# A linear attention and two feed-forward networks on one core: weight loads issued by ScalarE, attention rows moved within SBUF, a wait put off, empty products left out

## The reference

```python
# q, k, v, a_re, a_im: (B=4, H=8, S=768, D=48), float32
mag = sqrt(a_re**2 + a_im**2)
scale = minimum(mag, 0.999) / (mag + 1e-6)
for t in range(S):                       # a complex decay per head and column, a real state update
    S_re, S_im = ar*S_re - ai*S_im + k[t] (x) v[t],  ar*S_im + ai*S_re
    y[t] = q[t] @ S_re
x = y as (3072 tokens, 384)
xn = x / sqrt(mean(x*x) + 1e-6) * rms_g  # first network
x = (silu(xn @ w_gate) * (xn @ w_val)) @ w_out        # 384 -> 1536 -> 384
h = x @ w_in                             # second network
out = softplus(h) @ w_out2                            # 384 -> 2048 -> 384
```

## Time and profile before

| | |
|---|---|
| median of 3 runs | 1174.2 us (1171.81 to 1175.09) |
| the profiled execution | 1175.1 us, its span 1173.4 us |
| TensorE clock granted, mean | 0.997 of full speed |
| TensorE busy | 1074.7 us, 92% of the span |
| VectorE busy | 701.8 us, 60% |
| ScalarE busy | 679.3 us, 58% |
| GpSimd busy | 290.2 us, 25% |
| HBM read, written | 67.97 MB, 29.24 MB |
| `rows_scratch<-pk`, 24 stores of 771.0 KB | median 4.9 us to landing |
| `mm<-rows_scratch`, 96 loads of 192.8 KB | median 4.5 us to landing |
| `a_in`, 24 loads of 384.0 KB | median 4.9 us to landing |
| `kq_in`, 24 loads of 384.0 KB | median 5.9 us to landing |

### The profile page before, as it was taken

How to read it: one execution, slowest core, us unless ns; L and a number is a source line. 1 busy time by engine, 2 the same in 40 slices (tenths; PEclk the granted TensorE clock), 3 DMA queues, 4 the chain that set the end, 5 groups by cost and what they waited for, 6 DMA issues and landing times.

```text
span 1173.4 us, 17259 instructions
## 1 busy us (share of the span) xinstructions
PE 1074.7 (92%) x5495; PEld 913.2 (78%) x5495; DVE 701.8 (60%) x2227; ACT 679.3 (58%) x1217; POOL 290.2 (25%) x260
## 2 busy tenths in 40 slices
PE   0456689999999999999999999989999999999997
PEld 0456678888888888888888878878888888888886
DVE  7798959999999999999999211212221313122211
ACT  5566646555555565665554333466666667676664
POOL 2211211111111111111111116733333333333332
PEclk9999999999999999999999999989999999999999
DMA  4988853433343443334332303320100101010000
GB/s 114 208 206 216 189 128 88 115 89 88 89 137 100 106 132 107 88 88 116 88 89 75 101 1 122 119 70 1 52 3 1 55 0 54 0 54 0 27 1 28
DMA packets 69051, 98.15 MB, mean 84 GB/s; under 512 B 5232, under 2 KB 58864, under 8 KB 68976
## 3 DMA queue, kind: packets, MB, share of 16 engines
q1 hardware_dynamic: 63792, 90.15, 27.0%
q0 software_dynamic: 5184, 7.08, 3.9%
HBM read 67.97 MB, written 29.24 MB: 83 GB/s over the span
## 4 chain that ended last, share of the span: by engine, by line
PE 34%; issue 26%; DVE 11%; DMA 11%; POOL 10%; ACT 6%; SPq 1%; POOLq 0%; DVEq 0%; ACTq 0%
PE gbank L1488 16%; POOL pl L556 10%; PE ybank L1488 10%; DMA rows_scratch<-pk 5%; DMA mm<-rows_scratch 4%; DVE prep L882 3%; PE sbank L1505 2%; DVE pk L882 2%; PE xbank L1517 2%; PE xbank L1516 1%; PE xbank L1520 1%; ACT L730 1%; PE xbank L1496 1%; DMA ytile<-in_w 1%; DVE state L1066 1%
## 5 line engine op out<-in xcount | busy, mean ns | idle before, releaser
L1488 PE MATMUL gbank<-xh,slab 128*128 128x512 f32 x1296 | 404.3, 393 | 1.5 <-ACT xh L641 1.5
L1488 PE MATMUL ybank<-ph,slab 128*128 128x512 f32 x1020 | 319.6, 395 | 4.8 <-ACT ytile L678 3.9
L1488 PEld LDWEIGHTS gbank<-xh,slab 128*128 128x128 f32 x1296 | 241.5, 189 | 50.2 <-ACT xh L641 1.7
L1488 PE MATMUL gbank<-xl,slab 128*128 128x512 f32 x648 | 253.3, 391 | 0.0
L1488 PEld LDWEIGHTS ybank<-ph,slab 128*128 128x128 f32 x1020 | 189.3, 189 | 42.9 <-issue 5.6
L531 POOL TENSOR_TENSOR pl<-hid,ph 128x512 fp32r<-128x512 f32 x72 | 99.7, 1384 | 461.4 <-ACT ph L671 461.4
L1488 PE MATMUL ybank<-pl,slab 128*128 128x512 f32 x510 | 199.6, 391 | 0.0
L556 POOL TENSOR_TENSOR pl<-hid,ph 128x512 fp32r<-128x512 f32 x96 | 125.6, 1309 | 268.0 <-ACT ph L817 268.0
L1368 DVE SCALAR_TENSOR_TENSOR hid<-gbank,hid 128x512 f32<-128x512 f32 x72 | 49.7, 691 | 214.4 <-ACT hid L808 214.4
L1488 PEld LDWEIGHTS gbank<-xl,slab 128*128 128x128 f32 x648 | 122.0, 188 | 26.2
L1488 PEld LDWEIGHTS ybank<-pl,slab 128*128 128x128 f32 x510 | 96.2, 189 | 20.8
(11 more groups left out here) (155 smaller groups left out, 1604.0 us busy)
## 6 DMA issues: line engine op xcount, KB each, us to landing
rows_scratch<-pk SPq DMA_DIRECT2D x24, 771.0 KB, 4.9
mm<-rows_scratch SPq DMA_DIRECT2D x96, 192.8 KB, 4.5
a_in<-in_a SPq DMA_DIRECT2D x24, 384.0 KB, 4.9
kq_in<-in_kq SPq DMA_DIRECT2D x24, 384.0 KB, 5.9
ytile<-in_w SPq DMA_DIRECT2D x36, 192.0 KB, 4.7
slab<-in_w POOLq DMA_DIRECT2D x36, 192.0 KB, 5.7
prep<-in_w SPq DMA_DIRECT2D x32, 192.0 KB, 2.5
y_scratch<-ytile SPq DMA_DIRECT2D x7, 768.0 KB, 5.4
```

What stands on the lines that cost most here:

```text
L1488: last = pe.matmul(out, slab[:, slot + part, cols], x, start=f, stop=l)
```

## The change

1. **Rows within SBUF.** `rows_scratch`, `store_pk` and `load_mm` go. `move_rows(m, hf)` copies `pk` to `mm` by DMA from SBUF to SBUF: for each part z and each piece of a head that lies in one block of partitions, a DMA of 48, 32 or 16 rows of 257 numbers. A half has 5 pieces, so 10 DMAs, and a unit 20 (at most 48 x 257 numbers, 49 KB, each) instead of 1 + 4. `pk` is free when both halves have landed.
2. **SyncE's order.** In a lead step: ten moves, `load_v`, ten moves, `load_a(n+1)`, `load_kq(n)`. In a tile step `load_v` and ten moves, `load_a(n+1)`, ten moves, `load_kq(n)`.
3. **The first network's weight loads** are issued by ScalarE: those of block 0 at its start, and in `w1_hi(f)`, behind each kind's two copies, that kind of block f+1.
4. **ScalarE's order.** `w1_hi` of a lead step's first block stands between `front_sq(n+1)` and `front_ln(n+1)`; that of the second stays at the end.
5. **The late blocks' wait.** Before tile 0 TensorE waits for the weights of blocks 0 to 7; for those of 8 to 11 it waits in front of block 8 of tile 0.
6. **No empty products.** `out_block(0, 0)` and `out_block(0, 1)` return at once; the three opening matmuls close their groups and count `out_done` up by two.

```diff
+EARLY = 8
-        rows_d = nc.dram_tensor("rows_scratch", (2, 2, DM, ROW), F32, kind="Internal").ap()
...
-            def load_mm(m, hf, par):
-                after((pk_stored, 16 * (m + 1)), (ys_done[hf], m))
-                heads = slice(hf * HH, (hf + 1) * HH)
+            def move_rows(m, hf):
+                after((dprep.sem, dprep.at("Q", m)), (ys_done[hf], m))
                 for z in range(2):
-                    sp.dma_start(mm[z * D:(z + 1) * D, heads, :],
-                                 rows_d[par, z].rearrange("(h d) c -> d h c", d=D)[:, heads, :]).then_inc(
-                                     mm_loaded[hf], 16)
-
-            def store_pk(n, par):
-
-                after((dprep.sem, dprep.at("Q", n)))
-                sp.dma_start(rows_d[par].rearrange("z (j p) c -> p z j c", p=P), pk[:, :, :, :]).then_inc(pk_stored, 16)
-
-            def load_w1(f):
-                for kind in range(3):
-
-                    after((w_neg, 3 * f + kind + 1))
-                    sp.dma_start(stage1[:, kind, :], w1_d[f, kind]).then_inc(w_loaded[kind], 16)
+                    for h, d, j, p, rows in PIECES[hf]:
+                        sp.dma_start(mm[z * D + d:z * D + d + rows, h, :], pk[p:p + rows, z, j, :]).then_inc(mm_loaded[hf], 16)
...
-            def lead(n, m, par, w1):
+            def lead(n, m, par):
+                if m is not None:
+                    move_rows(m, 0)
+                    load_v(m)
+                    move_rows(m, 1)
                 load_a(n + 1)
-                if m is not None:
-                    load_v(m)
-                    load_mm(m, 0, 1 - par)
-                    load_mm(m, 1, 1 - par)
-                load_w1(w1[0])
                 load_kq(n)
-                load_w1(w1[1])
-                store_pk(n, par)
...
+            def load_w1(f, kind):
+                act.dma_start(stage1[:, kind, :], w1_d[f, kind]).then_inc(w_loaded[kind], 16)
...
                     act.activation(slab[:, 6 * f + 2 * kind + 1, :], slab[:, 6 * f + 2 * kind, :].bitcast(F32), ACT.Copy,
                                    scale=-1.0).then_inc(w_neg, 1)
+                    if f + 1 < F1:
+                        load_w1(f + 1, kind)
...
                 front_sq(n + 1)
+                w1_hi(w1[0])
                 front_ln(n + 1)
...
-                w1_hi(w1[0])
                 w1_hi(w1[1])
...
             def decay_column(n):
-                need(dve, pk_stored, 16 * n)
+                need(dve, mm_loaded[0], MOVED * n)
+                need(dve, mm_loaded[1], MOVED * n)
...
+                if T == 0 and f == EARLY and kind == 0:
+                    pe.wait_ge(w_hi, 3 * F1)
+                    pe.wait_ge(w_lo_late, 16 * 3 * (F1 - EARLY))
...
             def out_block(T, f):
+                if T == 0 and f < 2:
+                    return
...
-            pe.wait_ge(w_hi, 3 * F1)
-            pe.wait_ge(w_lo, 16 * 3 * F1)
+            pe.wait_ge(w_hi, 3 * EARLY)
+            pe.wait_ge(w_lo, 16 * 3 * EARLY)
...
+def pieces(hf):
+
+    out = []
+    for h in range(hf * HH, (hf + 1) * HH):
+        d = 0
+        while d < D:
+            c = h * D + d
+            rows = min(D - d, P - c % P)
+            out.append((h, d, c // P, c % P, rows))
+            d += rows
+    return out
+
+
+PIECES = [pieces(hf) for hf in range(2)]
+MOVED = 16 * 2 * len(PIECES[0])
```

More of the change, by code:

```diff
@@ L219, in program @@
         a_loaded, kq_loaded, v_loaded = sem("a_loaded"), sem("kq_loaded"), sem("v_loaded")
-        pk_stored, mm_loaded = sem("pk_stored"), [sem(f"mm_loaded{i}") for i in range(2)]
+        mm_loaded = [sem(f"mm_loaded{i}") for i in range(2)]
         afront, aprep = Stage(sem("act_front"), ACT_FRONT), Stage(sem("act_prep"), ACT_PREP)
@@ L229, in program @@
         w_loaded = [sem(f"w_loaded{i}") for i in range(3)]
-        w_hi, w_neg, w_lo = sem("w_hi"), sem("w_neg"), sem("w_lo")
+        w_hi, w_neg, w_lo, w_lo_late = sem("w_hi"), sem("w_neg"), sem("w_lo"), sem("w_lo_late")
         w2_loaded = [sem(f"w2_loaded{i}") for i in range(3)]
@@ L386, in step @@
                 if m is not None:
-                    load_mm(m, 1, 1 - par)
+                    move_rows(m, 1)
                 if n is not None:
                     load_kq(n)
-                if n is not None:
-                    store_pk(n, par)
             def store_y(T):
@@ L417, in _ @@
             sp.dma_start(mask_d, causal[:, :]).then_inc(mask_out, 16)
-            lead(0, None, 0, W1_LEAD[0])
+            lead(0, None, 0)
             sp.wait_ge(mask_out, 16)
@@ L422, in _ @@
             for n in range(1, LEAD):
-                lead(n, n - 1, n % 2, W1_LEAD[n])
+                lead(n, n - 1, n % 2)
             with sp.Fori(0, 2) as t:
@@ L518, in w1_lo @@
                     pool.dma_start(slab[:, 6 * f + 2 * kind + 1, :], w1_d[f, kind],
-                                   accum_op=ALU.add).then_inc(w_lo, 16)
+                                   accum_op=ALU.add).then_inc(w_lo if f < EARLY else w_lo_late, 16)
             def w2_lo_of(slot):
@@ L785, in _ @@
             act.preload_act_table_set(LN_EXP)
+            for kind in range(3):
+                load_w1(0, kind)
             act.wait_ge(const_ready, CONSTS)
@@ L1062, in decay @@
             def decay(m, hf):
-                dve.wait_ge(mm_loaded[hf], 32 * (m + 1))
+                dve.wait_ge(mm_loaded[hf], MOVED * (m + 1))
                 need(dve, s_added, 2 * m + hf - 1)
@@ L1491, in kt_of @@
             def kt_of(m, hf):
-                pe.wait_ge(mm_loaded[hf], 32 * (m + 1))
+                pe.wait_ge(mm_loaded[hf], MOVED * (m + 1))
                 need(pe, y_copied, 2 * m + hf)
@@ L1630, in _ @@
             pe.wait_ge(s_added, 2 * (LEAD - 1))
-            pe.wait_ge(w_hi, 3 * F1)
-            pe.wait_ge(w_lo, 16 * 3 * F1)
+            pe.wait_ge(w_hi, 3 * EARLY)
+            pe.wait_ge(w_lo, 16 * 3 * EARLY)
             pe.wait_ge(silu_done, 1)
             for m in range(NJ):
-                pe.matmul(ybank[m][:, :], slab[:, 0, 0:P], ph[:, 0, :], start=True, stop=False)
+                last = pe.matmul(ybank[m][:, :], slab[:, 0, 0:P], ph[:, 0, :], start=True, stop=True)
+            last.then_inc(out_done, 2)
             for T in range(NT):
```

## The result

The change takes **1206.6 us** (median of 4 runs, 1205.38 to 1207.57) against 1174.1 before it (4 runs): a ratio of 1.0275, 95% interval 1.0257 to 1.0292. It is slower by 32.5 us, where the forecast had 21; the time lies in the range (1182 to 1210). The profiled execution took 1207.6 us, its span 1205.8, with a mean granted clock of 0.993 (0.997 before). Two executions that were far slower than all others of their kernels, one of 2194 us of the kernel before and one of 6015 us of run 3, are left out of what follows.

What follows compares the result with a forecast made beforehand. It took the lead to be bound by VectorE's wait chain through two transfers, to HBM scratch and back. Lead +24.6, start +1, TensorE's start -2.2 and tile steps -2.4 gave +21.0 on 1174.2: 1195 us, range 1182 to 1210.

Steps and rivals of the forecast that it cites:

- The issue price: SyncE's queue in a lead step: each move or load issue holds it 0.46 us, bounds 0.41 and 0.66.
- `a_in`'s landing to the square: Lead step: from the issue of `a_in`'s load to ScalarE's square takes 4.6 us, bounds 3.5 and 5.0.
- `xh`: Lead step: ScalarE's new order delays `xh`, a new VectorE wait of 1.5 us before `lead_low`.
- The five: Lead steps after the opening one: 27.5 us, then four of 29.5, 145.5 against 120.9, so +24.6.
- The start: Kernel start: three weight loads compete with the first `a_in`, +1 us, bounds 0 and 2.9.
- TensorE's start of tile 0: After the lead: no wait for the last weight's low part, start set by VectorE's state, -2.2 us.
- Empty products: Tile 0: 4.1 us of TensorE work removed, but VectorE sets that point, 0 us, bounds 0 and -0.7.
- Tile steps: TensorE's five waits for `mm` go, `kq` comes in time: -2.4 us, bound 0.
- The low end: Whole kernel: issues of 0.41 on SyncE and 0.33 on ScalarE, landing 3.5: 1183 us, put at 1182.
- Rival A: Faster: moves leave SyncE almost without holding it, `load_a` bound by `load_v`'s wait; 1164 us, chance 0.10.
- the forecast: Lead: issues of 0.40 to 0.50 us and a late `a_in`; 1195 us, chance 0.80.
- C: Much slower: moves cost 0.66 us an issue, lead steps about 34.3 us; 1220 to 1250 us, chance 0.05.

Runs made afterwards that it cites:

- run 3: The change with rows again through the scratch in HBM (one store and four loads a unit, old order), all else kept: 1170.2 us, ratio 0.9959 to before.
- run 8: The change with the source of its 480 moves in HBM, same count, sizes and destination: 1189.7 us (one run).
- run 4: The change with moves of 129 instead of 257 columns, same number of DMAs: 1206.4 us (one run).
- run 6: Also called the mixture: the change with rows through the scratch, empty products kept, first three weight loads issued behind the first square: 1164.7 us, ratio 0.9914 to before.
- run 7: The kernel of run 6 with both weight blocks rounded at the end of ScalarE's lead step: 1173.0 us, ratio 0.9984 to before.
- run 9: The kernel of run 6 with TensorE waiting for all twelve blocks' weights before tile 0: 1164.8 us, ratio 0.9922 to before.
- run 5: The kernel before with only the empty products of tile 0 left out: 1177.5 us against 1174.95, ratio 1.0028.
- run 10: The kernel of run 6 with rows moved within SBUF from unit 5 on, in the tile steps alone: 1163.7 us, ratio 0.9911 to before.
- run 2: The change with `load_a` in the lead issued behind the first ten moves, ahead of the second ten: 1193.8 us, ratio 1.0171 to before.

## Why the prediction was right, and where its numbers were off

The verdict, the place and the mechanism were right: SyncE's queue holds `a_in` back, and `sum_of` waits for it. The size, +21 against +32.5, was off by terms that partly cancel, and it is in part by luck that the time lies in the range. With the measured issues alone, which bring `a_in` late by 18.9 us more over the five steps, the same sum gives 1195 + 18.9 = 1214, above the range (it allowed for 0.53 an issue and not for the upper bound of 0.66). Two terms that were too dear, the landing of `a_in` up to `sum_of` (6.5 us over the five steps) and the wait for `xh` (5.3), brought it back.

- **The issue price** (taken 0.46, bounds 0.41 and 0.66): 0.62 in the first ten of a step, 0.62 to 0.70 in the second, and 0.58 for the loads behind them. This is the step that failed. The reason given, "no store stands ahead of the moves", chose the lower of two rows. Both rows have their source in HBM, and for such a source the choice was right: the eight mask loads take 0.46 each in the change, where no store is ahead of them, and run 8 has 0.45. Half of the eight took under 0.47 before as well, and a few long ones, up to 1.27, made the mean. Runs 4 and 8 show that what costs more is a move with its source in SBUF, and not bytes or a store; no row of the kernel before had such a move. `a_in` was asked for at +14.1, not +9.7: 4.4 us late in that step.
- **`a_in`'s landing to the square** (taken 4.6): 77.52 - 73.84 = 3.7. It gave 0.9 back. That the scratch's traffic was gone is not what did it: in run 6 the rows go by the scratch, and `a_in` lands in 3.2 us in the lead (median; 4.6 before, 5.5 in run 7). Before the change and in run 7 the two blocks are rounded one right behind the other, in the change and in run 6 apart; no run varied the traffic of the weights alone.
- **`xh`** (a new wait of 1.5 each): 0.18. The step failed in charging ScalarE's three issues behind its copies; they run beside them. 1.3 back.
- Together: +4.4 - 0.9 - 1.3 = +2.2 on a step of 29.5, so 31.7, and that step took 31.5. In the others `a_in` is asked for at +13.2 to +13.6 and `sum_of` stands at +17.5 to +17.8, where I had +15.4; less the 1.3 that makes 30.4, and they took 30.4 to 30.8. The first, which has no `xh`, took 29.6 for 27.5. The five sum to 152.8 where I had 145.5: **+31.8 for +24.6**.
- **The start** (+1, bounds 0 and 2.9): +2.1. The first square stands at 7.45, not at 5.30 as in the earlier trace rows. Run 6, which issues the weight loads behind it, has it back at 5.31.
- **TensorE's start of tile 0** (-2.2): -2.6. The size was nearly right and the part it was put down to probably wrong: in the mixture the put-off wait is worth nothing (run 9), and ScalarE's earlier loads bring the start forward. In the change itself this was not tried.
- **Empty products** (0, bounds 0 and -0.7): a loss, +3.2 in the trace of the change and +2.5 in run 5. The step said that TensorE "would wait that much longer". It does, 3.65 us in one piece, and behind it comes the low clock. I had bounded that cost below by a gain and above by nothing: it had no row for a low clock, and it should have had a rival.
- **Tile steps** (-2.4, bound 0): -1.3. The waits on `mm` went as forecast, and `kq` was never late. TensorE's wait for the state is 5.2 us in 16 pieces, and takes part of the gain, as in run 10.

Two small slips in the working changed nothing. The low end's steps of 27.3 keep the wait of 1.5 although 0.33 an issue on ScalarE makes it 1.1, which gives 26.9 and a lead 1.6 us shorter. Rival A's first step is 22.3 by its own numbers, not 22.1.

Of the rivals, A (the moves leave SyncE unheld) is out by its own row: no move's issue was under 0.5 us. By its condition the forecast (issues of 0.40 to 0.50, chance 0.80) failed as well, and C (0.66, chance 0.05) was nearer. C yet gave 1220 and more, for it carried the same landing of 4.6 and the wait of 1.5, and charged the tile steps. The rule named in the prediction, from the Trainium skill, DMA: Bandwidth & Descriptors, section "Issuing engines are not separate DMA queues", that the sequencer time of a DMA is usually small relative to the DMA itself, is no guide in this lead. One issue of 0.6 us is still under a third of the 2.0 us to the move's landing, but twenty issues in a row take 12.4 to 13.3 us, and having ten of them ahead of one load costs 12.8 us (run 2).

## What to carry to other kernels

Count DMAs, not bytes, when a few large transfers are to be replaced by many small ones: multiply the count by an issue row with the same kind of source and destination, and ask what stands behind them in the same queue. Where the trace has no such row, let the range reach to the dearest row that it has. A change with several parts can hide a good one: here ScalarE's new order is worth 8 us beside its own weight loads, and the moves lose 36. Before work is taken from an engine that waits anyway, look at how long the idle piece becomes, and what the granted clock does behind it; work that seems useless may be what keeps TensorE's clock up.

## What the runs showed of the hardware that was not expected

- An issue on SyncE took 0.62 us with its source in SBUF and 0.45 with its source in HBM, for the same shape and destination (6.22 and 4.55 for ten, runs 4 and 8 beside the change), and 0.62 at half the bytes and for 16, 32 or 48 rows alike.
- A DMA issue on ScalarE took 0.33 to 0.34 us in the lead and ran beside the activation ahead of it: six copies took 2.9 us with three issues and 3.0 without.
- A TensorE idle of 3.65 us, behind a stretch at full clock, was followed by 5 us at a granted clock of 0.50 and 6 at 0.61 to 0.76 in the change and in run 5; in all six kernels with that idle the matmuls behind it took 9.9 to 11.2 us, and 7.4 in the six in which products of zeros filled it.
- The column PEclk is not all of the pace: the first 5 us of tile 0 read 1.00 in the change (187.80 to 193.10), yet its pairs of wide matmuls take 1.05 us there and 0.61 from 194.56 on. Before the change it is the same.
- The store of 771 KB took 4.7 us (median) to landing with the two blocks' weight traffic apart in the step (run 6), and 8.6 with both just ahead of it (run 7).
